# The second routing of a two-layer mixture-of-experts kernel: tokens as the stationary operand, x tiles loaded first, one group of twelve tiles, and plain writes for the sums

## The reference

```python
N, D, E, F = 1536, 512, 8, 1024          # tokens, width, experts, hidden width
skip_score = x @ w_skip                  # x: the output of the first mixture
do_compute = skip_score > 0
out = x.copy()
logits = xc @ w_gate                     # xc = x[do_compute]
e_idx = np.argmax(logits, axis=1)
probs = softmax(logits); gate_w = probs[row, e_idx]
for e in range(E):
    h = np.maximum(xc[mask] @ w1[e], 0.0)
    y[mask] = gate_w[mask, None] * (h @ w2[e])
out[do_compute] = xc + y
```

## Time and profile before

| | |
|---|---|
| median of 3 runs | 665.3 us (665.07 to 668.42) |
| the profiled execution's own time | 665.87 us |
| its span in the trace | 663.4 us |
| mean granted TensorE clock | 0.97 of full |
| TensorE busy | 620.8 us (94%) |
| VectorE busy | 367.9 us (55%) |
| ScalarE busy | 293.9 us (44%) |
| GpSimd busy | 237.9 us (36%) |

### The profile page before, as it was taken

How to read it: one execution, slowest core, us unless ns; L and a number is a source line. 1 busy time by engine, 2 the same in 40 slices (tenths; PEclk the granted TensorE clock), 3 DMA queues, 4 the chain that set the end, 5 groups by cost and what they waited for, 6 DMA issues and landing times.

```text
span 663.4 us, 13555 instructions
## 1 busy us (share of the span) xinstructions
PE 620.8 (94%) x4054; PEld 551.5 (83%) x4054; DVE 367.9 (55%) x714; ACT 293.9 (44%) x536; POOL 237.9 (36%) x223
## 2 busy tenths in 40 slices
PE   6888848999999999999999999998699999999994
PEld 6567735999999999999999999985478888888883
DVE  5759985644535554364644536423564687656641
ACT  2657732433424443253433434433255475646621
POOL 2558303105527063370725527033112223231230
PEclk9999967999999999999999999998699999999998
DMA  9999881442926448283672926885296679568220
GB/s 305 326 285 305 301 295 53 155 152 55 269 66 180 140 93 264 54 213 94 150 207 54 273 65 157 236 251 113 72 330 208 208 220 357 160 187 266 40 50 13
DMA packets 57633, 119.79 MB, mean 181 GB/s; under 512 B 13588, under 2 KB 13972, under 8 KB 57568
## 3 DMA queue, kind: packets, MB, share of 16 engines
q1 hardware_dynamic: 39424, 94.59, 43.4%
q0 software_dynamic: 14304, 23.93, 17.2%
q10 hardware_dynamic: 3840, 0.49, 0.5%
HBM read 103.51 MB, written 23.50 MB: 191 GB/s over the span
## 4 chain that ended last, share of the span: by engine, by line
PE 84%; DMA 5%; DVE 4%; issue 2%; SPq 2%; POOLq 0%; ACT 0%; POOL 0%; DVEq 0%; ACTq 0%
PE bank L964 22%; PE bank L856 22%; PE bank L850 22%; PE bank L839 2%; DMA q_ring<-in_q 2%; PE bank L819 2%; PE bank L745 2%; PE bank L980 2%; PE bank L724 1%; DMA xg<-x_moe,ix_take 1%; PE bank L768 1%; PE bank L758 1%; PE bank L713 1%; PE bank L936 1%; DVE col_val L1778 1%
## 5 line engine op out<-in xcount | busy, mean ns | idle before, releaser
L1615 DVE TENSOR_TENSOR w_lo<-stage,w_hi x120 | 141.7, 1222 | 22.9 <-ACT w_hi L1097 22.1
L1097 ACT CAST w_hi<-stage x120 | 119.7, 1050 | 9.0 <-PE bank L964 8.9
L856 PE MATMUL bank<-unit_hi,w_hi 128*128 128x416 f32 x256 | 92.6, 362 | 0.0
L1873 DVE SCALAR_TENSOR_TENSOR unit_lo<-bank,unit_hi 128x416 fp32r<-128x416 f32 x64 | 37.9, 592 | 96.8 <-ACT unit_hi L1211 96.8
L850 PE MATMUL bank<-tok_hi,w_hi 128*128 128x416 f32 x256 | 90.5, 354 | 0.6 <-DVE tok_lo L1825 0.6
L1211 ACT ACTIVATE unit_hi<-bank 128x416 fp32r<-128x416 f32 x64 | 33.2, 519 | 129.9 <-PE bank L850 129.9
L856 PE MATMUL bank<-unit_lo,w_hi 128*128 128x416 f32 x256 | 90.2, 352 | 0.0
L850 PE MATMUL bank<-tok_hi,w_lo 128*128 128x416 f32 x256 | 89.7, 350 | 0.0
L856 PE MATMUL bank<-unit_hi,w_lo 128*128 128x416 f32 x256 | 89.7, 350 | 0.0
L1429 POOL DMA_INDIRECT x_more<-more_out,ix_put x32 | 51.6, 1614 | 42.2 <-DVE more_out L1844 26.3
L1441 POOL DMA_INDIRECT x_moe<-rows_out,ix_put x32 | 55.2, 1726 | 9.8 <-issue 9.8
(11 more groups left out here) (162 smaller groups left out, 1072.5 us busy)
## 6 DMA issues: line engine op xcount, KB each, us to landing
stage<-in_moe_w SPq DMA_DIRECT2D x128, 512.0 KB, 5.6
v_win<-in_v SPq DMA_DIRECT2D x24, 198.0 KB, 8.9
v_raw<-in_v SPq DMA_DIRECT2D x6, 528.0 KB, 13.4
x_moe<-rows_out SPq DMA_DIRECT2D x12, 260.0 KB, 3.6
kt<-in_k SPq DMA_DIRECT2D x8, 384.0 KB, 9.0
q_ring<-in_q SPq DMA_DIRECT2D x6, 512.0 KB, 9.6
x_att<-x_sb POOLq DMA_DIRECT2D x12, 256.0 KB, 5.8
x_part<-x_moe SPq DMA_DIRECT2D x4, 768.0 KB, 8.8
```

The costliest lines, as they stand in the source:

```text
L856: last = eng.matmul(ps_out[chunk][:, 0:W], w[:, WC // 2 + f, chunk * P:(chunk + 1) * P], h[:, f % UNITS, :], start=(f == 0 and i == 0), st ...
L1097: eng.copy(piece(w_hi[n % SETS], j), stage[:, j, :]).then_inc(s_hi, 1)
L1615: eng.tensor_tensor(piece(w_lo[n % SETS], j), stage[:, j, :], piece(w_hi[n % SETS], j).bitcast(F32), ALU.subtract)\
L1873: eng.scalar_tensor_tensor(unit_lo[:, f % UNITS, :], ps_unit[f % 2][:, 0:W], 0.0, unit_hi[:, f % UNITS, :].bitcast(F32), ALU.max, ALU.subt ...
```

## The change

In the loop the transposed tile becomes the stationary operand and `wgate2` the moving one, so that the logits come out as 128x9 in their final place, in one bank for all twelve tiles; the turn of the result, its copies on ScalarE, their buffer and their semaphores go. SyncE issues all twelve tile loads first, and the wait for the sums and the load of `more_logit` after them. The second routing has one group of twelve tiles; ScalarE makes the `lane_hot` of tiles 1, 3, 5, 7, 9 and 11. After the loop TensorE issues 32 transposes of the identity ahead of `ranks`. The scatter of `more_out` is a plain write in every round. ScalarE stores the gates in one DMA.

```diff
-        GROUPS = (((0, NT),), ((0, NT // 2), (NT // 2, NT)))
+        GROUPS = (((0, NT),), ((0, NT),))
-        by_act = [2 * t + 1 for t in range(NT)] + [2 * NT + t for t in range(GROUPS[1][1][0], NT, 2)]
+        by_act = [2 * t + 1 for t in range(NT)] + [2 * NT + t for t in range(1, NT, 2)]
         def second_place(t0, t1):
-            ps = bank[5] if t0 < GROUPS[1][0][1] else bank[4]
-            return ps[:, t0 * (E + 1):t1 * (E + 1)]
+            return bank[5][:, t0 * (E + 1):t1 * (E + 1)]
             for t in range(NT):                                   # SyncE
-                if t == NT - 1:
-                    all_rounds = eng.snap(total, min_val=1, max_val=E * ROUNDS)
-                    for part in range(PARTS):
-                        eng.wait_ge(s_put_sums[part], all_rounds * 16)
-                    eng.dma_start(more_logit[:], more_dram.rearrange("(p t) e -> p t e", t=NT))\
-                       .then_inc(s_more, 16)
                 if t >= XR:
                     eng.wait_ge(s_x1t, t - XR + 1)
                 eng.dma_start(x1_sb[:, t % XR, :], ...)
+            all_rounds = eng.snap(total, min_val=1, max_val=E * ROUNDS)
+            for part in range(PARTS):
+                eng.wait_ge(s_put_sums[part], all_rounds * 16)
+            eng.dma_start(more_logit[:], more_dram.rearrange("(p t) e -> p t e", t=NT)).then_inc(s_more, 16)
             def second_logits(t):                                 # TensorE
-                if t >= 2:
-                    eng.wait_ge(s_gte, t - 1)
                 for i in range(DK):
-                    last = eng.matmul(gt_place(t)[0:E + 1], wgate2[:, i, :], xt_b[t % 2][:, i, :],
-                                      start=(i == 0), stop=(i == DK - 1))
-                last.then_inc(s_gt[1], 1)
-            def turn_logits(t):
-                eng.wait_ge(s_gte, t + 1)
-                eng.transpose(second_place(t, t + 1), gt_sb[:, t % 2, :],
-                              ident[0:E + 1, 0:E + 1]).then_inc(s_gl, 1)
+                    last = eng.matmul(second_place(t, t + 1), xt_b[t % 2][:, i, :], wgate2[:, i, :],
+                                      start=(i == 0), stop=(i == DK - 1), skip_group_check=True)
+                last.then_inc(s_gl, 1)
-            first, second = GROUPS[1]
-            for t in range(NT + 2):
+            for t in range(NT + 1):
 ...
-                if t == first[1] + 4:
-                    ranks(1, first)
-                if 1 <= t <= NT:
+                if t:
                     eng.wait_ge(s_x1te, t)
                     second_logits(t - 1)
-                if t >= 2:
-                    turn_logits(t - 2)
-            lists(1, first)
-            ranks(1, second)
-            lists(1, second)
+            keep_busy(32, ps_turn)
+            for group in GROUPS[1]:
+                ranks(1, group)
+                lists(1, group)
             def empty_x1(t):                                      # ScalarE
-                    eng.wait_ge(s_gt[1], t - 1)
+                    eng.wait_ge(s_gl, t - 1)
-            for t in range(NT + 1):
-                if t < NT:
-                    empty_x1(t)
-                if t:
-                    empty_gt(t - 1)
-                if t == first[1] + 3:
-                    weights(1, first)
+            for t in range(NT):
+                empty_x1(t)
+            weights(1, GROUPS[1][0])
             eng.wait_ge(s_m1done, 1)
-            store_gates(1, first)
-            weights(1, second)
-            store_gates(1, second)
-            lanes(1, second)
+            store_gates(1, GROUPS[1][0])
+            lanes(1, GROUPS[1][0])
                                                more_out[0:rows, t, :], None, bounds_check=N - 1,   # GpSimd
-                                               oob_is_err=False, compute_op=ALU.add)\
-                           .then_inc(s_put_sums[t], 16)
+                                               oob_is_err=False).then_inc(s_put_sums[t], 16)
```

More of the change, by code:

```diff
@@ L306, in build @@
         col_f = sb_in(routing, "col_f", [P, 2, NT])
-        gt_sb = sb_in(routing, "gt_sb", [E + 1, 2, P])
         XR = PARTS
@@ L359, in build @@
         s_xst = [sem(f"s_xst{i}") for i in range(2)]
-        s_gt = [sem(f"s_gt{m}") for m in range(2)]
+        s_gt = sem("s_gt")
         s_z = sem("s_z")
@@ L376, in build @@
         s_route = sem("s_route")
-        s_gte = sem("s_gte")
         s_gl = sem("s_gl")
@@ L484, in empty_job @@
                 if job[1] >= 2:
-                    eng.wait_ge(s_gt[0], job[1] - 1)
+                    eng.wait_ge(s_gt, job[1] - 1)
                 dst, src = xt_a[job[1] % 2][:], ps[:].rearrange("p (i n) -> p i n", i=DK)
@@ L497, in piece @@
             return buf[:].rearrange("p (j c) f -> p j (c f)", c=PC)[:, j, :]
-        GROUPS = (((0, NT),), ((0, NT // 2), (NT // 2, NT)))
+        GROUPS = (((0, NT),), ((0, NT),))
         group_no = {mg: i for i, mg in enumerate((m, g) for m in range(2) for g in GROUPS[m])}
-        by_act = [2 * t + 1 for t in range(NT)] + [2 * NT + t for t in range(GROUPS[1][1][0], NT, 2)]
+        by_act = [2 * t + 1 for t in range(NT)] + [2 * NT + t for t in range(1, NT, 2)]
         block = keep.enter_context(nc.Block())
-        def gt_place(t):
-            return bank[3 - t % 2][:, 0:P]
         def second_place(t0, t1):
-            ps = bank[5] if t0 < GROUPS[1][0][1] else bank[4]
-            return ps[:, t0 * (E + 1):t1 * (E + 1)]
+            return bank[5][:, t0 * (E + 1):t1 * (E + 1)]
         @block.sync
@@ L760, in router_logits @@
                                       skip_group_check=True)
-                last.then_inc(s_gt[0], 1)
+                last.then_inc(s_gt, 1)
             def second_logits(t):
-                if t >= 2:
-                    eng.wait_ge(s_gte, t - 1)
                 for i in range(DK):
-                    last = eng.matmul(gt_place(t)[0:E + 1], wgate2[:, i, :], xt_b[t % 2][:, i, :],
-                                      start=(i == 0), stop=(i == DK - 1))
-                last.then_inc(s_gt[1], 1)
-            def turn_logits(t):
-                eng.wait_ge(s_gte, t + 1)
-                eng.transpose(second_place(t, t + 1), gt_sb[:, t % 2, :],
-                              ident[0:E + 1, 0:E + 1]).then_inc(s_gl, 1)
+                    last = eng.matmul(second_place(t, t + 1), xt_b[t % 2][:, i, :], wgate2[:, i, :],
+                                      start=(i == 0), stop=(i == DK - 1), skip_group_check=True)
+                last.then_inc(s_gl, 1)
             def ranks(m, group):
@@ L1128, in _ @@
                         empty_job(eng, job)
-            eng.wait_ge(s_gt[0], NT)
+            eng.wait_ge(s_gt, NT)
             noise_scale(NT - TAIL, NT)
@@ L1172, in empty_x1 @@
                 if t >= 2:
-                    eng.wait_ge(s_gt[1], t - 1)
+                    eng.wait_ge(s_gl, t - 1)
                 eng.copy(xt_b[t % 2][:], ps_x1[t % 2][:].rearrange("p (i n) -> p i n", i=DK))\
                    .then_inc(s_x1te, 1)
-            def empty_gt(t):
-                eng.wait_ge(s_gt[1], t + 1)
-                if t >= 2:
-                    eng.wait_ge(s_gl, t - 1)
-                eng.copy(gt_sb[:, t % 2, :], gt_place(t)[0:E + 1]).then_inc(s_gte, 1)
             def first_mixture():
```

## The result

The changed kernel takes 673.3 us (median of 4 runs, 672.17 to 674.31), and the kernel before took 665.7 us beside it (4 runs, 665.07 to 668.42): a ratio of 1.0107, with a 95% interval of 1.0068 to 1.0146. The forecast was 661.3 with a range up to 663.7. The changed kernel is 1.1% slower, and what came is the rival to which the prediction gave 0.06, the clock's fall in the loop. In this document a ratio leaves out the executions that lie over 1.5% above the fastest one of the same kernel (only e8 has any, four of twelve); a median keeps them.

What follows compares the result with a forecast made beforehand. TensorE held 84% of the chain, but the gain lay in the second routing: routing start 457.2 plus 10.7 put `take_ix` at 467.9 against 471.94, 4.0 us less. From 665.3 that gave 661.3 us, range 659.6 to 663.7.

Steps and rivals of the forecast that it cites:

- the clock's fall in the loop: Rival: nine moving columns count as idleness, TensorE drops to 1.2 GHz in the tile loop; up to 670.8 us; chance 0.06.
- Part 1: Tile loop on TensorE: with tokens standing, a step takes 1.38 us instead of 1.71; last logits at 457.1.
- T: Moment VectorE can start a routing that has all twelve tiles: forecast 457.2, against 464.66 before for the last six.
- Part 2: Tile loads first: tile 11's load of 4.7 us is hidden, and `more_logit` lands at 456.2, 0.9 us under 457.1.
- the late load: Rival: tiles 9 to 11 or `more_logit` come late among the row puts, costing 1 to 2.5 us; chance 0.22.
- Part 3: Second routing as one group of twelve: 10.7 us to `take_ix` instead of 7.28, from width, lists and identity transposes.
- Part 4: ScalarE's one store of the gates: its wait costs nothing, with some 1.7 us of cover.
- Part 5: Plain scatter writes: save 0 to 2.3 us of GpSimd's time each round, off the path; taken as nothing.
- The named harm: With plain writes the rows' puts meet the loads of tiles 8 to 10, up to 2.3 us earlier.
- Part 6: Behind the index table: gather issued 1.34 us later, all moves with it; slow first slot taken as nothing, bound 1.2 us.

Runs made afterwards that it cites:

- e8: The changed kernel with the add back in the scatter of `more_out`: 673.4 us, ratio 1.0097.
- e1: The kernel before with only the new form of the logits (tokens standing, nine columns moving), nothing else changed: 666.1 us, ratio 1.0004.
- e2: The changed kernel with the old form of the logits (tokens moving, with the turn and its copies): 667.1 us, ratio 1.0014.
- e3: The changed kernel with four more identity transposes in each loop step from tile 3 on: 666.4 us, ratio 1.0029.
- e6: The changed kernel with the nine moving columns repeated fourteen times in the same instruction (126 columns): 666.1 us, ratio 1.0024.
- e13: The changed kernel with 126 moving columns and plain writes, the same program as e6 in a later batch: 664.0 us, ratio 0.9984.
- e7: The changed kernel with the nine moving columns repeated seven times (63 columns): 671.4 us, ratio 1.0114.
- e9: The changed kernel with 126 moving columns and 8 identity transposes behind the loop instead of 32: 667.1 us, ratio 1.0026.
- e15: The changed kernel with 126 moving columns, plain writes and no identity transposes behind the loop: 663.9 us, ratio 0.9979.
- e10: The changed kernel with 126 moving columns and the add back in the scatter of the sums: 662.6 us, ratio 0.9980.
- e16: The same as e11 but without the identity transposes behind the loop: 660.5 us, ratio 0.9939.
- e14: The changed kernel with 126 moving columns and the add back, e10 again in a later batch: 662.3 us, ratio 0.9950.
- e12: The kernel before, unchanged, profiled a second time: the index table came 29.1 us behind the first copy, not 31.3.
- e4: The changed kernel without the 32 identity transposes behind the loop: 668.8 us, ratio 1.0064.
- e11: e10 with SyncE's copy of the base rows into `out` waiting for the second gather too: 661.1 us, ratio 0.9951.
- e5: The changed kernel run again, unchanged: 674.8 us, ratio 1.0147.

## Why the prediction was wrong

- **Part 1, the step's work: right, its clock: wrong.** 1.28 us at full clock against 1.38 forecast. The step that failed is the assumption under parts 1 and 3 that the clock stays at 1.00 until the ranks are done, with a chance of 0.06 for the rival. "Nine columns against 16 I cost alike" was a statement about durations and was true; I let it stand for the clock as well. The row called against the rival, attention's clock of 1.00 with 16 and 65 moving columns, was taken from a mixture in which groups of that form alternate with others, not from a loop that is little else. e1, e2, e3 and e6 show the cause.
- **Its price.** From the first copy to T the forecast had 16.6 us (440.65 to 457.2), and it took 26.0 (439.40 to 465.36). Of the 9.4 more, six steps of tiles 6 to 11 give 6.0 (447.89 to 462.15 is 14.3, against 6 x 1.38), the last sixteen matmuls 1.4 (3.21 against 1.78), and the hold-up 2.4, a part of which is itself the slow clock; the faster early steps give back 0.4. The rival's own price for slow steps, 0.8 each, was too small: a step rose by 1.2 (2.46 against 1.28), for everything in a step slows down: four transposes take 0.95 for 0.49, eight logit matmuls 1.51 for 0.80. Its price for the 32 transposes, 3.1, was too large: they took 5.80, 2.3 more than 3.5. That the rival's 670.8 lies near the measured 673.3 is in part luck, since it has no hold-up in it.
- **Part 2, the loads: right in order, wrong in size with plain writes.** VectorE's wait in L1644 was for TensorE, not for `more_logit`, and the trace of the changed kernel names no late tile. At full clock the late load came true with plain writes: 1.37 us in e13, near the 1.5 us worked out for a load of 6.4, and 0.20 to 1.50 in e6, e7, e9 and e15.
- **Part 3.** `mask_b` 2.2 us behind T (forecast 2.5), and from the ranks' product to the table 6.46 (forecast 6.4): the width and the lists were sized rightly. The wait for the ranks was 2.6 instead of 0.8, from the transposes at 1.2 GHz; at full clock it is 0.26 (e10). 12.6 us in sum against 10.7. At full clock it takes 10.3 (e10, 456.54 to 466.87) and 10.0 without the block (e16).
- **Part 4: right.** ScalarE's first `lane_hot` started at 473.08, waiting for `lane_f` and not for the store.
- **Part 5: right in kind, wrong in sum.** A plain put of the sums takes GpSimd 1.04 us where the one with the add took 1.61; nobody waited for that time. The named harm, the rows' puts meeting the tile loads, was taken as nothing and is what e13 shows against e14.
- **Part 6: right.** The gather was issued 1.32 us behind the table, and the second mixture took 0.6 us more than before, inside the bound of 1.2. TensorE's wait for the second gather was 1.27 us for 0.56; it was 1.36 in the second profile of the kernel before (e12), so it takes no change to see it.
- **The yardstick.** Even with the clock held and the add back, the change brings 0.2 to 0.5% (e10 and e14), 1.6 to 3.3 us, not 4.0, and e10's interval still reaches 1.0007: the single profile of before held a stall that its second profile has not.

**What stays open.** The hold-up at tiles 3 to 5 was in five of eight profiles with plain writes and short steps (the changed kernel twice, e6, e7, e9; not in e4, e13, e15) and in none of six with the add (e1, e8, e10, e11, e14, e16). e6 and e13 are the same program, one with it and one without, so it is a matter of the single execution, perhaps made likelier by the plain writes. In e5, e6, e7 and e9 the trace names what TensorE waits for: ScalarE's copy of tile 4 (2.06, 1.33, 1.38 and 2.03 us); in the changed kernel's first profile it puts the same pause down to "issue". Why the copy starts late is open. That the hold-up brings the clock down sooner is not shown: with nine columns the fall came 6.5 and 9.6 us behind the first copy with it (after, e5), and 5.6, 6.9 and 9.6 us without it (e8, e1, e4). With 126 columns the clock survived it in e6 and fell behind it in e9.

## What to carry to other kernels

When an operand swap leaves a loop with full weight loads and a few moving columns, ask for the granted clock of such a loop and not only for the duration of its instructions; a row from a mixed stretch is no evidence. If the clock falls, repeating the few columns in the same instruction (here 9 to 126, for 0.05 us a step) can be cheaper than filler in between, and filler behind the loop comes too late and stands in the way. And measure the stretch in a second profile of the kernel before, before you count a stall there as yours to win.

## What the runs showed of the hardware

- **The clock.** TensorE fully busy by the trace, with 128-column weight loads, four 128-column transposes and eight matmuls of 9 columns a step, was granted 0.50 (1.2 GHz) in five profiles of four kernels (the changed one twice, e1, e4, e8). With 126 columns in the same instructions it was granted 1.00 in seven (e6, e10, e11, e13 to e16), and in an eighth, e9, it dipped only behind an idle stretch. The Trainium skill, "TensorE: Matmul & The Clock Gate", tells of a clock lost in DMA waits (HAM oscillation) and in small idle times between groups of matmuls (A second HAM failure mode: psum-queue depth-cycling). This case's trace shows a fall with no idle time in the records (e1, 446 to 450).
- **Transposes.** Four extra transposes a step held the clock (e3), and it came back during the 32 transposes (468 to 472 after). The Trainium skill, on the same page (Part 4: PE-mode transpose), says that the full clock doesn't engage for transposes; the measurement speaks against it for these, which the trace records as matmuls.
- **A scatter with and without the add.** A plain indirect scatter of 36-byte rows cost GpSimd 1.04 us against 1.61 with the add, and the page of the profile counts 11,488 packets in its queue instead of 14,304 for the same 23.93 MB. The Trainium skill, "DMA: Bandwidth & Descriptors" (Specifications), says that below 512 B the engine does a read-modify-write; the landing times, 3.4 us (e13) and 3.9 (e14) for one put each, neither bear that out nor refute it.
- **The spread.** Runs of one program in one batch differ by 7.6 us (the kernel before: 661.8 to 669.4) and by 9.0 (e15: 661.5 to 670.5), so an edit worth 2 us is hard to tell from none: the interval takes in 1.0 in eight of the table's fifteen rows.
